# The opening of a fused attention, routing and MLP kernel: the first head's k and q loaded once and doubled on the chip, proj's load moved, and unread products on TensorE up to the first scores

## The reference, cut to what matters

```
q_bits = (q @ proj > 0); k_bits = (k @ proj > 0)          # 6 bits for each row
mask   = bucket(q_bits)[:, None] == bucket(k_bits)[None, :]
scores = where(mask, q @ k.T / sqrt(64), -1e9)             # 2 x 8 heads, 768 rows, 64 columns
x      = softmax(scores) @ v                               # then rows of 512 for 1536 tokens
x      = moe(x, w_gate, w1, w2)                            # 8 experts, 192 tokens each, greedy routing
out    = silu(x @ w_in) @ w_out                            # 512 -> 2048 -> 512
```

## Time and profile before

| what | value |
|---|---|
| median of 3 runs | 822.85 us (822.58 to 825.09) |
| the profiled execution | 823.09 us |
| its span, first to last instruction | 821.3 us |
| TensorE busy with matrix products | 792.1 us, 96% of the span |
| VectorE / ScalarE / GpSimd busy | 63% / 33% / 12% |
| mean granted TensorE clock | 0.99 of full speed |

### The profile page before, as it was taken

One profiled execution on the slowest core, in us unless ns is written; L12 is line 12 of the kernel. 1 busy time (PEld: TensorE's weight loads), 2 busy tenths in 40 slices (PEclk: granted clock), 3 DMA queues, 4 the chain that ended last, 5 costly groups with the idle time before them and its releaser, 6 DMA issues.

```text
span 821.3 us, 14817 instructions
## 1 busy us (share of the span) xinstructions
PE 792.1 (96%) x5538; PEld 644.2 (78%) x5543; DVE 514.5 (63%) x1215; ACT 269.7 (33%) x578; POOL 102.5 (12%) x140
## 2 busy tenths in 40 slices
PE   5899999999999988999999999999999999999996
PEld 4666676676766645899999999998888788878885
DVE  5888888888888798887779774074332433343331
ACT  3565666666666611212212221231112111131101
POOL 4111212312122311011011000000000100010001
PEclk9999999999999999899999999999999999999999
DMA  6132514325152105353545437720000100010001
GB/s 136 40 77 46 131 49 101 93 48 131 36 114 55 36 20 174 124 186 131 179 155 163 173 129 280 282 106 1 1 1 0 51 0 0 0 51 0 0 0 51
DMA packets 74603, 68.79 MB, mean 84 GB/s; under 512 B 52288, under 2 KB 60480, under 8 KB 73536
## 3 DMA queue, kind: packets, MB, share of 16 engines
q1 hardware_dynamic: 70976, 60.82, 25.0%
q0 software_dynamic: 2240, 7.34, 2.8%
q10 hardware_dynamic: 1344, 0.04, 0.1%
HBM read 61.90 MB, written 6.29 MB: 83 GB/s over the span
## 4 chain that ended last, share of the span: by engine, by line
PE 92%; DVE 3%; issue 1%; ACT 1%; DMA 1%; POOL 1%; ACTq 0%; DVEq 0%; POOLq 0%
PE pt_ps L1473 16%; PE score_ps L1456 15%; PE pt_ps L1357 11%; PE pt_ps L1369 10%; PE pt_ps L1240 8%; PE pv_ps L1202 5%; PE score_ps L1190 4%; PE score_ps L1202 4%; PE score_ps L1191 4%; PE work_ps L1300 3%; PE score_ps L1163 1%; PE work_ps L1163 1%; PE score_ps L1345 1%; PE pt_ps L1378 1%; PE score_ps L1290 1%
## 5 line engine op out<-in xcount | busy, mean ns | idle before, releaser
L1473 PE MATMUL pt_ps<-y_s,w_in_s 128*128 128x512 f32 x576 | 137.8, 390 | 2.7 <-DVE y_s L1118 2.0
L1456 PE MATMUL score_ps<-w_out_s,gate_s 128*128 128x512 f32 x576 | 137.4, 389 | 0.0
L1473 PEld LDWEIGHTS pt_ps<-y_s,w_in_s 128*128 128x128 f32 x576 | 107.9, 188 | 26.2 <-DVE y_s L1118 2.8
L1456 PEld LDWEIGHTS score_ps<-w_out_s,gate_s 128*128 128x128 f32 x576 | 108.1, 188 | 22.4
L1136 DVE TENSOR_TENSOR gate<-pt_ps,sig 128x512 f32<-128x512 f32 x48 | 33.2, 691 | 146.4 <-ACT sig L629 146.4
L505 ACT ACTIVATE att_area<-att_area 128x768 f32<-128x768 f32 x96 | 90.0, 937 | 91.1 <-DVE att_area L837 91.1
L837 DVE TENSOR_SCALAR_CACHE_REDUCE att_area<-score_ps 128x768 f32<-128x768 f32 x96 | 91.8, 956 | 22.2 <-PE score_ps L1191 20.9
L1357 PE MATMUL pt_ps<-area,experts_w 128*128 128x192 f32 x512 | 98.3, 340 | 1.5 <-ACT area L589 1.2
L629 ACT ACTIVATE sig<-pt_ps 128x512 f32<-128x512 f32 x48 | 28.7, 598 | 210.5 <-PE pt_ps L1473 210.5
L1369 PE MATMUL pt_ps<-area,experts_w 128*128 128x192 f32 x512 | 87.2, 328 | 0.0
L1357 PEld LDWEIGHTS pt_ps<-area,experts_w 128*128 128x128 f32 x512 | 83.6, 193 | 2.1 <-ACT area L589 2.1
(11 more groups left out here) (203 smaller groups left out, 1019.5 us busy)
## 6 DMA issues: line engine op xcount, KB each, us to landing
experts_w<-in_moe_w SPq DMA_DIRECT2D x16, 2048.0 KB, 8.6
experts_w<-in_k SPq DMA_DIRECT2D x16, 384.0 KB, 4.2
experts_w<-in_q SPq DMA_DIRECT2D x16, 384.0 KB, 5.1
experts_w<-in_moe_w_in SPq DMA_DIRECT2D x8, 512.0 KB, 4.8
w_out_raw<-in_moe_w_out SPq DMA_DIRECT2D x4, 1024.0 KB, 8.6
att_area<-in_v SPq DMA_DIRECT2D x16, 192.0 KB, 2.4
x_rows<-att_area SPq DMA_DIRECT2D x8, 384.0 KB, 3.1
area<-x_rows,ids_now POOLq DMA_INDIRECT x16, 4.0
```

The source lines that it names most:

```text
L1456: done = nc.tensor.matmul(out_ps[m], gate_s[:, fo % RING_S, a, m * P:(m + 1) * P], w_out_s[:, fo, b, :], start=(fo == 0 and a + b == 0), s ...
L1473: done = nc.tensor.matmul(layer_ps[f % 2][:, 0:GT], w_in_s[:, a, w_cols], y_s[:, c, b, :], start=(c == 0 and a + b == 0), stop=(c == DC - ...
```

## The change

- SyncE loads k and q of head 0 with each row written once, into columns 0 to 63 of each block. ScalarE copies k into columns 64 to 127, VectorE copies q. TensorE waits for a new semaphore for each copy before it turns k and q.
- ScalarE's two loads of proj come ahead of its first Exp. `bit_proj` and `ones` are set by VectorE, as its first two memsets, and no longer by GpSimd.
- `keep_busy` is moved up and takes the bank as an argument. TensorE now runs 13 such products of 512 columns as soon as `ones` is there, 3 after the transposes of q, 4 before the scores of tile 0, 3 between the scores of tiles 0 and 1, and 3 after those of tile 1. They write the upper half of `score_ps[1]`. The calls in the routing stage keep their counts and their bank.

```
--- before.py
+++ after.py
@@ -231,6 +231,8 @@
         s_zeros = sem("zeros_ready")
         s_step_c = sem("const_step")
         s_proj_zero = sem("proj_zeroed")
+        s_ones = sem("ones_ready")
+        s_doubled = sem("first_rows_doubled")
         s_proj = sem("proj_loaded")
         s_wg = sem("w_gate_loaded")
         s_gate_zero = sem("gate_cols_zeroed")
@@ -399,7 +401,8 @@
                 sp.dma_start(v_nat[p], head(v_rows, h)).then_inc(s_v[p], 16)
 
             sp.sem_inc(s_xw, 16)
-            load_qk(0, 0)
+            for rows, nat, loaded in ((k_rows, k_nat, s_k), (q_rows, q_nat, s_q)):
+                sp.dma_start(nat[0][:, :, 0:D], head(rows, 0)).then_inc(loaded[0], 16)
             sp.wait_ge(s_proj, 32)
             load_v(0, 0)
             load_qk(1, 1)
@@ -481,13 +484,15 @@
 
         @block.scalar
         def _(act):
-            act.wait_ge(s_const, 1)
-            nc.scalar.activation(row_sum[:, 0:1], ident[:, 0:1], ACT.Exp)
             act.wait_ge(s_proj_zero, 1)
             proj_twice = proj.unsqueeze(1).broadcast_to([D, 2, BITS])
             for r0 in (0, D):
                 twice = bit_proj[r0:r0 + D, D:P].rearrange("d (r c) -> d r c", r=2)[:, :, 0:BITS]
                 act.dma_start(twice, proj_twice).then_inc(s_proj, 16)
+            act.wait_ge(s_const, 1)
+            nc.scalar.activation(row_sum[:, 0:1], ident[:, 0:1], ACT.Exp)
+            act.wait_ge(s_k[0], 16)
+            nc.scalar.activation(k_nat[0][:, :, D:P], k_nat[0][:, :, 0:D], ACT.Copy).then_inc(s_doubled, 1)
 
             def drain_work(kind, half, w, high, p_next, bank=work_ps):
 
@@ -646,7 +651,6 @@
             step(nc.gpsimd.memset(ident[:, :], 0.0))
             nc.gpsimd.affine_select(out=ident[:, :], in_=ident[:, :], compare_op=ALU.not_equal, fill=1.0,
                                     base=0, pattern=[[-1, P]], channel_multiplier=1).then_inc(s_const, 1)
-            nc.gpsimd.memset(bit_proj, 0.0).then_inc(s_proj_zero, 1)
             nc.gpsimd.memset(to_x[:, :, P:DE], 0.0).then_inc(s_gate_zero, 1)
             pool.sem_inc(s_logits, 1)
             for shift, upper, lower in ((q_shift, 0.0, -1.0), (k_shift, BIG, 0.0)):
@@ -663,7 +667,6 @@
                 step(nc.gpsimd.memset(after[:, :], 1.0))
                 step(nc.gpsimd.affine_select(out=after[:, :], in_=after[:, :], compare_op=ALU.is_gt, fill=0.0,
                                              base=0, pattern=[[-1, P]], channel_multiplier=1))
-                step(nc.gpsimd.memset(ones[:, :], 1.0))
                 small = dict(allow_small_or_imprecise_dtypes=True)
                 step(nc.gpsimd.iota(e_rank[:, :], pattern=[[-1, E]], base=E, channel_multiplier=0, **small))
                 step(nc.gpsimd.iota(left[:, :], pattern=[[-1, E]], base=E, channel_multiplier=0, **small))
@@ -884,8 +887,13 @@
                 nc.vector.scalar_tensor_tensor(tie_0[:, same], best_row_0[:, same], best[:, i:i + 1], after[:, :],
                                                ALU.is_equal, ALU.mult).then_inc(s_tie, 1)
 
+            nc.vector.memset(bit_proj, 0.0).then_inc(s_proj_zero, 1)
+            nc.vector.memset(ones[:, :], 1.0).then_inc(s_ones, 1)
             for rows in (high_alone, low_alone, k_bits[0], k_bits[1]):
                 nc.vector.memset(rows[D:P, :].bitcast(f32), 0.0).then_inc(s_zeros, 1)
+            dve.wait_ge(s_doubled, 1)
+            dve.wait_ge(s_q[0], 16)
+            nc.vector.tensor_copy(q_nat[0][:, :, D:P], q_nat[0][:, :, 0:D]).then_inc(s_doubled, 1)
             dve.wait_ge(s_const, 2)
             for i in range(PREP):
                 drain_work(PREP_KINDS[i], i % 2, i, i, 0, bank=first_banks[i % 4])
@@ -1205,14 +1213,28 @@
                 if b == T - 1:
                     done.then_inc(s_pv, 1)
 
+            def keep_busy(n, bank, cols=512):
+
+                for _ in range(n):
+                    nc.tensor.matmul(bank[:, 0:cols], ones[:, :], ones[:, 0:1].broadcast_to([P, cols]),
+                                     start=True, stop=True)
+
+            pe.wait_ge(s_ones, 1)
+            keep_busy(13, pv_banks[1])
             pe.wait_ge(s_const, 1)
             for i in range(PREP):
-                if i == 4:
+                if i in (0, 2):
+                    pe.wait_ge(s_doubled, 1 + i // 2)
+                elif i == 4:
+                    keep_busy(3, pv_banks[1])
                     pe.wait_ge(s_proj_step, 6)
                     pe.wait_ge(s_zeros, 4)
                 fill_work(PREP_KINDS[i], i % 2, FIRST_NEEDS[i] or None, 0, 0, 0, first_banks[i % 4])
+            keep_busy(4, pv_banks[1])
             scores(0, 0, PREP, 0)
+            keep_busy(3, pv_banks[1])
             scores(1, 0, PREP, 1)
+            keep_busy(3, pv_banks[1])
 
             def row_of_first_batch(w):
 
@@ -1332,7 +1354,7 @@
                                                 token_id[:, j, :],
                                                 start=(j == 0 and k == 0), stop=(j == NT - 1), skip_group_check=True)
                     if r == 0:
-                        keep_busy(1, 256)
+                        keep_busy(1, layer_ps[0], 256)
                 done.then_inc(s_perm, 1)
 
             def turn_rows(r, k):
@@ -1372,27 +1394,21 @@
 
             FIRST_PARTS = [[2], [3, 4], [5], [6, 7], [8], [9, 10], [11]]
 
-            def keep_busy(n, cols=512):
-
-                for _ in range(n):
-                    nc.tensor.matmul(pt_ps[0][:, 0:cols], ones[:, :], ones[:, 0:1].broadcast_to([P, cols]),
-                                     start=True, stop=True)
-
-            keep_busy(3)
+            keep_busy(3, layer_ps[0])
             row_of_second_batch()
-            keep_busy(4)
+            keep_busy(4, layer_ps[0])
             pe.wait_ge(s_wants, 1)
...
```

More of the change, by code:

```diff
@@ L1386, in _ @@
                 rank_part(0, i)
-                keep_busy(4 if T - 1 <= i < NT - 1 else 0)
+                keep_busy(4 if T - 1 <= i < NT - 1 else 0, layer_ps[0])
             rank_ties(0)
-            keep_busy(4)
+            keep_busy(4, layer_ps[0])
             count(0)
-            keep_busy(7)
+            keep_busy(7, layer_ps[0])
             token_of_slot(0)
-            keep_busy(5)
+            keep_busy(5, layer_ps[0])
             row_of_best(1)
-            keep_busy(12)
+            keep_busy(12, layer_ps[0])
             turn_rows(0, 0)
```

11 lines of the change are left out of this document (6 added, 5 removed).

## The result

| | before | changed |
|---|---|---|
| median of 14 runs, us | 823.63 (822.37 to 826.82) | 820.20 (818.08 to 822.71) |
| ratio, 95% interval | | 0.9954 (0.9941 to 0.9966) |
| the profiled execution, us | 823.09 | 820.74 |
| its span, us | 821.3 | 819.0 |
| first scores start at, us | 12.72 | 11.10 |

The change is 3.4 us faster, 0.46%. The page of the changed kernel has the same shape as before; TensorE is on the chain for 91% instead of 92.

What follows compares the result with a forecast made beforehand. TensorE was taken to bound the kernel (92% of the chain), with the opening setting the first scores' start. Earlier scores (-0.34) and later third scores (+0.09) sum to -0.25 us: median 822.6, eight-in-ten range 821.0 to 824.1.

Steps and rivals of the forecast that it cites:

- The landing of k: Opening: k's halved load, issued at 0.89, lands between 3.4 and 4.96 us, taken as 4.2.
- the order of events at the 13 products: Ahead of k's transposes: k is ready at 4.7 us, so the products, not the load, set the first transpose.
- the formula for their end: 13 products from 1.35 us, 0.43 each until the clock rises at 5.2, then 0.22: first transpose at 6.07.
- The landing of proj: Opening: proj's second load, issued 0.63 us earlier at 1.85, lands between 5.25 and 6.15 us.
- The products behind the second scores: Three products after scores 1 don't quite fit TensorE's wait: third scores 0.09 us later.
- From there to the scores: First transpose at 6.07 to first scores at 12.38, 0.34 us earlier than before, VectorE's eight operations running without a gap.
- The clock comes up at once and stays: Rival, opening and attention: rise at 4.8, scores 0.57 earlier, the fall at 29.7 gone for 1.0 more; 821.4, chance 0.20.
- the third rival: Between 7.5 and 12 us the clock falls again before the scores are under way: 1.0 us lost, 823.6, chance 0.12.
- The loads and the copies are irrelevant: Opening: they are hidden behind the products, and undoing them alone should move nothing much; no separate chance given.
- VectorE's two gaps: Before the first scores VectorE starved 0.64 us because q landed late and 0.58 us because proj landed late.
- a shift of the first scores passes to the end one to one: Whole kernel: whatever moves the first scores moves everything behind by the same amount, here 0.34 us earlier.
- My own sign of being wrong: Products ending well before k, first scores before 11.8 or after 13.3, or the time moving more than the first scores.

Runs made afterwards that it cites:

- the twenty profiles: All the study's profiles; of ten with the groups of 3, 4, 3 and 3 products nine show no fall in attention, of ten without them eight show one.
- the undone loads: The change with k and q of head 0 loaded doubled as before, without the two copies: 821.22 us, 0.9977 of the kernel before.
- a delay of 1.1 us: The change with 12 products instead of 4 ahead of the first scores: 823.52 us, 0.9990 of the kernel before.
- guards: Products added in TensorE's waits near 26 us and at routing's ranks and second count; 818.30 us on the change with 10 first products, 823.18 on the kernel before.

## Why the prediction was wrong

**Right.** The landing of k, the start of the copies, the order of events at the 13 products and the formula for their end: the first transpose comes at 5.74 with the clock up at 4.6 instead of 5.2, and at 6.44 and 6.66 with the rises at 6.1 and 6.5 in the other two profiles. The landing of proj was right by luck: I expected it from the issue 0.63 us earlier, and it came from the halved loads ahead of it (5.20; with halved loads and the late issue 5.34, with doubled loads and the early issue 6.96). The products behind the second scores cost nothing (third scores 4.03 after the first; 4.02 before).

**The step that failed first** is "From there to the scores": "Its eight operations follow without a gap", at 0.64 each, and "ScalarE's copies come 0.64 apart". I took the 0.64 from the rows of before for VectorE's own pace. It was TensorE's: at the low clock three transposes take 0.66 and the two products of a bits half 2 x 0.32, as TensorE's timeline of the kernel before shows:

```profile
5.65 0.85 PE L1163 MATMUL pt_ps<-ident,experts_w 128*128 128x128 f32 x3
...
9.79 0.52 PE L1165 MATMUL pt_ps<-k_high,proj_mixed 128*128 128x384 f32 x1
10.11 0.52 PE L1166 MATMUL pt_ps<-k_bits,high_alone 128*128 128x384 f32 x1
10.43 0.52 PE L1169 MATMUL pt_ps<-q_parts,proj_high 128*128 128x384 f32 x1
```

At the high clock VectorE's own pace shows, 0.47 to 0.53 between its last six operations, and ScalarE's 0.38. The term was 6.31 and measured 5.36; alone it moves the first scores from 12.38 to 11.43, the earlier rise of the clock in the first profile to 11.10. It is worth 0.95 us, and the forecast with it corrected, 821.65, would still have been 1.4 too high, but inside the range. The steps that follow put the time outside.

**The second** is the rival "The clock comes up at once and stays", to which I gave 0.20 and against which I wrote that "nothing in the change shortens that wait". The wait is as long as before (1.67 us), but the fall behind it was absent in all three profiles of the change and present in two of three of the kernel before. Nothing shortened the wait; the products of the short groups, which I had priced only as cover for TensorE's waits, kept the fall away, as the twenty profiles say. The sum held nothing for it, and it measured 1.2 us between first scores and attention's last minimum (272.4 against 271.3 on average). The Trainium skill, TensorE: Matmul & The Clock Gate, Part 1, says that the low start is "run-variable", the same kernel having 6, 11 or 14 slow matmuls. The change agrees: 8, 11 and 12 of its 13 products ran slow in its three profiles. The rule on transposes, which I had weighed as the third rival, isn't borne out as a loss: no profile of a kernel with all the opening's products has a fall between the transposes and the scores.

**The third** is the last rival, "The loads and the copies are irrelevant. That is my forecast for them". By the medians they are most of the gain: 0.9966 alone, against 0.9989 for the products alone. I had looked only at what stands ahead of k's first transpose, where the products do hide k's copy, and priced q's and proj's loads at nothing. VectorE's two gaps, which I had named as bounding the opening, come from these two loads landing late. Landing early removes them without delay (first transpose 4.98, scores 11.39); the products alone remove them only by starting later (6.66, 12.25). Behind the products the undone loads cost 1.0 us in the medians, less than these can tell. That the two gaps explain all that the medians give the loads isn't shown, since the two kernels stand level at the end of attention.

**The fourth** is the assumption that a shift of the first scores passes to the end one to one and is all that counts. Through attention it does pass so. In the medians it doesn't: a delay of 1.1 us cost 3.3. Over three profiles each the change is 2.1 us ahead at the end of attention, 0.9 by the shift and 1.2 by low clock behind it; the medians say 3.4. My own sign of being wrong, a time that moves by more than the first scores do, came true.

**What stays open** is the remaining 1.3 us. The profiled executions don't hold it: they average 822.9 and 821.6, 1.3 apart and not 3.4. The medians don't follow the start either. Eight kernels without guards have their first scores between 10.41 and 12.05, and medians from 820.07 to 821.22 in no order of the start; three and the kernel before have them between 12.25 and 12.85, and medians from 823.04 to 823.63. It looks like a step near 12.1, of which the profiles show no cause. The runs' clocks say that low stretches are fewer: 0.991 on average over 98 runs of the kernel before, 0.994 over the change's 14. A difference of 0.003 over 820 us is 2.5 us, one and a half stretches of 3.4 us at half clock, or 1.6 us at 1.1 each. But the profiles of the part behind attention don't show it, and the guards, which raised the clock of the kernel before to 0.996, gave it at most 0.8 us. Why the same guards give 1.9 to 2.2 us behind the early start and not behind the late one was not settled. Also open is the worth of the 13 products. The kernels without them have their first scores between 11.19 and 11.63, the change between 11.10 and 12.03, so they move the start by nothing that shows; 10 instead of 13 gave 10.41 and 10.24.

## What to carry to other kernels

When an engine's operations follow each other evenly, ask whose pace it is before it goes into a sum: here VectorE's 0.64 us was two slow matmuls of TensorE, and changed with the clock. Look at several executions, and at every variant that has or lacks a piece of code, before a fall of the clock is put down to the kernel or to chance; if the runs of one kernel spread by 4 us, profile it three times. Smaller loads ahead of a serial opening can be worth more than the bytes say, since everything queued behind them, here proj, lands early without being moved.

## What the runs showed of the hardware

- A stretch of low clock lasted 3.4 us (twice that in some places) and cost about 1.1 us: the change's two runs at 0.989 average 822.5, its five at 0.996 average 818.8; 0.007 of 818 us is 3.4 stretches at half clock for 3.7 us. In attention one cost 0.8 to 1.1 us, read from the profiles. The clock isn't all: among the 35 runs of the kernel before on one chip, those with a mean clock of 0.993 took 820.75 to 826.22 us.
- VectorE's copy of 384 columns took 0.36 us inside SBUF (5.08 above), against 0.56 for its operations that read the matmul results; ScalarE's took 0.52 against 0.49.
- ScalarE's table load took 1.28 us in both places, and its DMA issues ahead of it held it back until 2.58, with no effect on k's copy, which waited for the load.
- Halving the bytes of k and q, with a 256-byte piece each as before, brought q's landing from 6.8 to 5.1 and left the issue on SyncE's queue nearly as long (0.73 for k and 0.64 for q, against 0.78 and 0.84).
- proj's two loads of 3 KB landed with the bytes ahead of them. Its split began at 5.05 to 5.40 with 192 KB each of k and q, and at 6.74 to 7.05 with 384 KB each, in all twenty profiles and whether proj was first issued at 1.1 or at 1.7 us.
